# Selection flags of two row tiles side by side: three block turns a pair and a second indicator table

## What is computed

```
ub = sum(max(q * k_min, q * k_max))        # per query and chunk, chunks past the query masked
top_chunks = argsort(ub)[..., -6:]
scores = q @ k.T / 8                       # kept where the key's chunk is in top_chunks and key <= query
attn = softmax(scores);  x = attn @ v
```

## Time and profile before

| | |
|---|---|
| median of three runs | 276.93 us |
| the profiled execution | 276.81 us, its span 274.6 us |
| PE | 264.2 us busy, 96% of the span, 3630 matmuls |
| POOL | 223.4 us, 81% |
| DVE | 208.0 us, 76% |
| ACT | 151.2 us, 55% |

### The profile page before, as it was taken

The page is one execution under the profiler, slowest core; times in us unless marked ns, Lnnn a source line. Parts: engine busy times, 40 slices in busy tenths (PEclk is TensorE's granted clock), DMA queues, the critical chain, the costliest instruction groups (busy, mean ns, idle before and its releaser), DMA issues.

```text
span 274.6 us, 8756 instructions
## 1 busy us (share of the span) xinstructions
PE 264.2 (96%) x3630; PEld 167.8 (61%) x3630; DVE 208.0 (76%) x565; ACT 151.2 (55%) x228; POOL 223.4 (81%) x297
## 2 busy tenths in 40 slices
PE   7899999999999999999999999999999999987994
PEld 7556666565666565666665656757565657664663
DVE  5895787486969989758879897899799978962342
ACT  2295656565666565646584546465756576851220
POOL 6077999999999999998999999989899971726832
PEclk9999999999999999999999999999999999999999
DMA  9999999998999999999799979999998979511861
GB/s 149 181 151 145 272 207 168 328 195 168 180 183 178 171 175 182 171 174 184 128 188 169 202 129 196 155 200 175 181 345 189 299 167 201 106 40 50 156 137 62
DMA packets 154838, 48.31 MB, mean 176 GB/s; under 512 B 142447, under 2 KB 144358, under 8 KB 154768
## 3 DMA queue, kind: packets, MB, share of 16 engines
q1 hardware_dynamic: 141728, 28.73, 52.2%
q0 software_dynamic: 9936, 18.64, 38.6%
q10 hardware_dynamic: 3136, 0.39, 0.9%
HBM read 55.46 MB, written 11.01 MB: 242 GB/s over the span
## 4 chain that ended last, share of the span: by engine, by line
PE 89%; DVE 3%; ACT 2%; DMA 1%; issue 1%; another core or an unknown queue 1%; ACTq 1%; POOL 0%; DVEq 0%
PE OB L611 27%; PE SC L534 26%; PE SC L553 6%; PE OB L1357 4%; PE SC L1331 4%; PE MM L647 4%; PE OB L693 3%; PE MM L624 2%; PE MM L500 2%; PE SC L474 2%; PE MM L474 2%; DMA qn<-in_q_dram 1%; ACT EXB L562 1%; PE MM L686 1%; PE SC L794 1%
## 5 line engine op out<-in xcount | busy, mean ns | idle before, releaser
L562 ACT ACTIVATE EXB<-SC 128x1024 f32<-128x1024 f32 (+1 forms) x87 | 83.1, 966 | 38.4 <-PE SC L534 25.3
L586 POOL TENSOR_TENSOR ES<-ES,EXB 128x256 f32<-128x256 f32 (+1 forms) x98 | 96.9, 999 | 4.7
L534 PE MATMUL SC<-qT,kT 64*128 64x512 f32 (+3 forms) x476 | 86.3, 465 | 0.4 <-ACT EXB L562 0.3
L611 PE MATMUL OB<-EXB,vn 128*64 128x256 f32 (+3 forms) x704 | 72.6, 361 | 0.0
L611 PEld LDWEIGHTS OB<-EXB,vn 128*64 128x64 f32 x704 | 46.8, 137 | 23.1 <-issue 9.7
L534 PEld LDWEIGHTS SC<-qT,kT 64*128 64x128 f32 x476 | 39.3, 187 | 20.2 <-issue 14.5
L586 POOL TENSOR_TENSOR ES<-EXB 128x512 f32<-128x512 f32 (+1 forms) x29 | 45.2, 1560 | 2.4
L572 POOL TENSOR_SCALAR_AFFINE_SELECT EXB<-EXB 128x256 f32<-128x256 f32 x79 | 34.7, 450 | 3.8 <-ACT EXB L562 3.8
L619 ACT ACTIVATE oT<-OB 128x512 f32<-128x512 f32 (+1 forms) x32 | 15.7, 490 | 40.2 <-PE OB L611 40.2
L553 PE MATMUL SC<-unsT,ind 64*128 64x256 bf16 (+5 forms) x238 | 35.6, 295 | 0.0
L553 PEld LDWEIGHTS SC<-unsT,ind 64*128 64x128 bf16 x238 | 11.7, 94 | 18.5 <-issue 9.5
(11 more groups left out here) (266 smaller groups left out, 400.8 us busy)
## 6 DMA issues: line engine op xcount, KB each, us to landing
w1s<-in_moe_w_dram POOLq DMA_DIRECT2D x8, 1024.0 KB, 10.1
w2s<-in_moe_w_dram POOLq DMA_DIRECT2D x7, 1024.0 KB, 9.5
vn<-in_v_dram SPq DMA_DIRECT2D x32, 192.0 KB, 3.2
kn<-in_k_dram SPq DMA_DIRECT2D x62, 96.0 KB, 2.8
qn<-in_q_dram SPq DMA_DIRECT2D x62, 96.0 KB, 7.3
out_dram<-w1s SPq DMA_DIRECT2D x2, 1536.0 KB, 10.7
x_rows<-xp SPq DMA_DIRECT2D x16, 192.0 KB, 3.3
out_dram<-out_dram SPq DMA_DIRECT2D x1, 1536.0 KB, 12.2
```

The source lines that it names most:

```text
L534: op("pe", lambda: pe.matmul(o, kT[j][pr, ts(kt)], qT[j][pr, q0:q1], start=not flags and (not cols or cols[0] == 0), stop=bool(flags)), r= ...
L562: op("act", lambda: ac.activation(Ex(st, None, 0, W), src, ACTF.Exp, scale=SCALE), r=pk, w=[f"E{st}"])
L586: op(e, lambda: sy.queue[e].tensor_tensor(o, in0, in1, ALU.add), r=[f"E{s2}", f"E{first[0]}"] if first else [f"E{s2}"] + kt, w=kt)
L611: op("pe", lambda: pe.matmul(OB[pr, q0:q1], vn[s][:, kt, h, :], ex, start=(n == 0), stop=last), r=[f"vn{s}{h}", "ES0" if st is None else f ...
```

## The change

The flags of two row tiles stand side by side in one block. Within each head's 64 columns of a block, columns 0 to 23 hold a tile of queries 128 to 511, and columns 32 to 55 a tile of queries 512 to 767. So three blocks are turned instead of five, ACT copies 384 columns instead of 640 (for pair 0 in one copy instead of two), and DVE makes the flags in two comparisons, of three and of two tiles.

In the turned flags, queries from 512 on lie 32 partitions lower. Their product therefore needs a table whose rows are moved by 32: `ind2`, zero but for rows 32 to 63 of each half, which two transfers on SP copy from `ind`, one for each half. A piece of the triangle that crosses query 512 gets two products for each head instead of one. Three of the eight pieces do.

```diff
-                uns = al(pers, "uns", [128, NT - 1, 2, D], BF16)
-                unsT = [al(pers, "unsT", [128, (NT - 1) * 128], BF16) for _ in range(2)]
+                uns = al(pers, "uns", [128, NT // 2, 2, D], BF16)
+                unsT = [al(pers, "unsT", [128, NT // 2 * 128], BF16) for _ in range(2)]
...
+                ind2 = al(pers, "ind2", [128, NT * 128], BF16)
...
-                    return bass.AP((uns, unsT[0])[fb - 6], 0, [[(NT - 1) * 2 * D, 128], [1, Dm]])
+                    return bass.AP((ind, ind2)[fb - 6], 0, [[NT * 128, 128], [1, Dm]])
...
+                op("dve", lambda: ve.memset(ind2[:], 0.0), w=["ind2"])
...
-                    op("dve", lambda: ve.tensor_tensor(un, uv, thr, ALU.is_lt),
-                       r=["ubm", "M0"] + [f"top{t}{h}" for t in range(NT - 1) for h in range(2)], w=["uns"])
+                    for t0, n, half in ((0, NT // 2, 0), (NT // 2, NT // 2 - 1, 1)):
...
+                        un = bass.AP(uns, half * 32, [[NT // 2 * 2 * D, 128], [D, 2], [2 * D, n], [1, NCH]])
...
+                        op("dve", lambda: ve.tensor_tensor(un, uv, thr, ALU.is_lt),
...
-                    for t in range(NT - 1):
+                    for t in range(NT // 2):
...
-                    for c0, c1, key in ((0, 384, f"unsT{j}"), (384, (NT - 1) * 128, "unsTb")) if i == 0 else ((0, (NT - 1) * 128, f"unsT{j}"),):
-                        op("act", lambda: ac.activation(unsT[j][:, c0:c1], MB[:, c0:c1], ACTF.Copy), r=["MB"], w=[key])
+                    op("act", lambda: ac.activation(unsT[j][:], MB[:, 0:NT // 2 * 128], ACTF.Copy), r=["MB"], w=[f"unsT{j}"])
...
-                                op("pe", lambda: pe.matmul(o, ind[pr, ts(kt)], unsT[j][pr, b0 - 128:q1 - 128],
-                                                           start=early, stop=not early),
-                                   r=[f"ind{h}", f"unsT{j}"] + (["unsTb"] if i == 0 and st else []), w=pk, inc=last and not early)
+                            segs = [(lo, hi, t, n) for lo, hi, t, n in ((b0, min(q1, S // 2 + 128), ind, 0), (max(b0, S // 2 + 128), q1, ind2, 1)) if lo < hi]
+                            for g, (s0, s1, it, half) in enumerate(segs):
+                                for h in range(2):
...
+                                    m = 128 + half * (S // 2)
+                                    op("pe", lambda: pe.matmul(o, it[pr, ts(kt)], unsT[j][pr, s0 - m:s1 - m],
+                                                               start=early and g == 0, stop=not early and g == len(segs) - 1),
+                                       r=[f"ind{h}", f"indB{h}", f"unsT{j}"] if half else [f"ind{h}", f"unsT{j}"], w=pk,
...
                 load(2, "qk")
                 unselT(0)
                 score_mm(0, 2, None, (256, 512))
+                for h in range(2):
+                    op("sp", lambda: sp.dma_start(ind2[h * 64 + 32:h * 64 + 64, :], ind[h * 64:h * 64 + 32, :]), r=[f"ind{h}", "ind2"], w=[f"indB{h}"],
+                       dsem=f"d_ind{h}")
                 take_q(1)
                 take_k(1)
                 load(3, "qk")
```

More of the change, by code:

```diff
@@ L490, in bounds_out @@
                                r=["ubm"], w=[f"top{t}{h}"], inc=(t == NT - 2 and h == 1))
-                    thr = bass.AP(top8, 5, [[(NT - 1) * 16, 128], [8, 2], [16, NT - 1], [0, NCH]])
-                    un = bass.AP(uns, 0, [[(NT - 1) * 2 * D, 128], [D, 2], [2 * D, NT - 1], [1, NCH]])
-                    uv = bass.AP(MM, 192, [[1024, 128], [160, 2], [32, NT - 1], [1, NCH]])
-                    op("dve", lambda: ve.tensor_tensor(un, uv, thr, ALU.is_lt),
-                       r=["ubm", "M0"] + [f"top{t}{h}" for t in range(NT - 1) for h in range(2)], w=["uns"])
+                    for t0, n, half in ((0, NT // 2, 0), (NT // 2, NT // 2 - 1, 1)):
+                        thr = bass.AP(top8, 5 + t0 * 16, [[(NT - 1) * 16, 128], [8, 2], [16, n], [0, NCH]])
+                        un = bass.AP(uns, half * 32, [[NT // 2 * 2 * D, 128], [D, 2], [2 * D, n], [1, NCH]])
+                        uv = bass.AP(MM, 192 + t0 * 32, [[1024, 128], [160, 2], [32, n], [1, NCH]])
+                        op("dve", lambda: ve.tensor_tensor(un, uv, thr, ALU.is_lt),
+                           r=["ubm", "M0"] + [f"top{t}{h}" for t in range(NT - 1) for h in range(2)], w=[f"uns{half}"] + (["uns"] if half == 0 else []))
                 def unselT(i):
                     j = i % 2
-                    for t in range(NT - 1):
+                    for t in range(NT // 2):
                         op("pe", lambda: pe.transpose(MB[:, ts(t)], uns[:, t, :, :].rearrange("p a b -> p (a b)"), ident_bf[:]),
-                           r=["uns", "ident_bf"], w=["MB"], inc=(t == NT - 2))
-                    for c0, c1, key in ((0, 384, f"unsT{j}"), (384, (NT - 1) * 128, "unsTb")) if i == 0 else ((0, (NT - 1) * 128, f"unsT{j}"),):
-                        op("act", lambda: ac.activation(unsT[j][:, c0:c1], MB[:, c0:c1], ACTF.Copy), r=["MB"], w=[key])
+                           r=["uns", "uns0", "uns1", "ident_bf"], w=["MB"], inc=(t == NT // 2 - 1))
+                    op("act", lambda: ac.activation(unsT[j][:], MB[:, 0:NT // 2 * 128], ACTF.Copy), r=["MB"], w=[f"unsT{j}"])
                 def mid(i):
@@ L549, in scores @@
                             assert not early or b0 == q0
-                            for h in range(2):
-                                pr = slice(h * 64, h * 64 + 64)
-                                o = ps[:, pb + h * 512 + c + b0 - q0:pb + h * 512 + c + q1 - q0]
-                                op("pe", lambda: pe.matmul(o, ind[pr, ts(kt)], unsT[j][pr, b0 - 128:q1 - 128],
-                                                           start=early, stop=not early),
-                                   r=[f"ind{h}", f"unsT{j}"] + (["unsTb"] if i == 0 and st else []), w=pk, inc=last and not early)
+                            segs = [(lo, hi, t, n) for lo, hi, t, n in ((b0, min(q1, S // 2 + 128), ind, 0), (max(b0, S // 2 + 128), q1, ind2, 1)) if lo < hi]
+                            for g, (s0, s1, it, half) in enumerate(segs):
+                                for h in range(2):
+                                    pr = slice(h * 64, h * 64 + 64)
+                                    o = ps[:, pb + h * 512 + c + s0 - q0:pb + h * 512 + c + s1 - q0]
+                                    m = 128 + half * (S // 2)
+                                    op("pe", lambda: pe.matmul(o, it[pr, ts(kt)], unsT[j][pr, s0 - m:s1 - m],
+                                                               start=early and g == 0, stop=not early and g == len(segs) - 1),
+                                       r=[f"ind{h}", f"indB{h}", f"unsT{j}"] if half else [f"ind{h}", f"unsT{j}"], w=pk,
+                                       inc=last and not early and g == len(segs) - 1)
                             if early:
```

## The result

The changed kernel takes 290.86 us (median of 6 executions, 287.58 to 292.89) where the kernel before takes 276.88 on the same chip: a ratio of 1.043, with an interval of 1.035 to 1.050. The prediction was 285.0 with a range of 282.4 to 287.0. Direction and first cause were right, the size was not: 3 us are missing in the profiled execution, which took 287.89 us (span 285.6), and 3 more between that one and the median. The runs come from several chips, so each kernel is compared with the kernel before on its own chip.

A forecast was written before the change was run, and what follows sets the result against it. PE, busy 96% of the span and gapless from pair 1 on, was taken as the bound. Turns -1.7, split couples +0.2, wait +7.6 and clock +2.1 give +8.2 us on 276.81: 285.0, range 282.4 to 287.0.

The forecast's parts named there:

- The wait: PE in pair 0 waits for both table copies, queued on SP behind pair 2's loads: 8.1 us, net 7.6.
- The clock: After the wait in pair 0 PE's clock is at half speed for some microseconds: 2.1 us lost (1.4 to 2.9).
- Rival 2: Pair 0's wait alone costs time; the clock stays up or comes back at once: 282.9 us, chance 0.14.
- The split couples: Three more couples of products a pair on PE, same columns streamed: 0.2 us in all, upper end 4.5.
- Rival 3: Each split couple on PE costs a gap, 4.5 instead of 0.2 us in all: 289.3 us, chance 0.05.
- The turns: Two fewer turns a pair on PE save 0.115 us a pair, 1.7 us over 15 pairs; pair 0 gives nothing.
- rival 4: POOL or DVE becomes the bound, so PE's saving is not had: 286.5 us, chance 0.09.
- from pair 1 on, PE should again be gapless: Expected sign in the changed trace: after pair 0 PE runs without gaps, each pair about 0.1 us shorter.

The follow-up runs named there:

- The kernels with the copies elsewhere: Changed kernel with wide useless products at the start and the copies behind pair 3's loads (285.91 us, 1.045), ahead of the v loads (279.64 us, 1.019) or behind them (277.09 to 285.73).
- the kernel kept at work: Changed kernel with 36 more useless products of 512 columns ahead of the couple that waits for the copies: 284.15 us, 1.024 of the kernel before.
- the one with early copies: Changed kernel with the two table copies issued ahead of the v loads instead of behind pair 2's loads: 281.66 to 291.05 us in four executions.
- the shifted kernel before: Kernel before with 20 of its 62 useless start products replaced by 84 of 32 columns, 128 more PE instructions: 282.96 to 290.13 us in four executions.
- the kernel with early copies and wide useless products: Changed kernel with the copies ahead of the v loads and 16 useless start products of 512 columns for 62 of 128: 279.64 us, 1.019.

## Why the prediction was off

- **The wait: right.** Copies issued at 18.83 and 19.49 us (forecast 18.43 and 19.0), read at 21.02 and 21.43, 2.2 and 1.9 us later (forecast 2.4, and 21.4 for the second). The wait, 8.1 us by the forecast, is 7.7 us to the first copy and 8.1 to the second. First values 9.44 us late against 7.6 + 2.1 = 9.7. The kernels with the copies elsewhere bear out the place in the queue as the cause.
- **The clock: right.** 2.1 us forecast, 1.8 by the kernel kept at work. The step used the trace's own fall at the end and its rise at the start (5.8 us for 53 products is 0.109 us each, not 0.107, which changes nothing). Rival 2, the wait alone, falls: the granted clock was 0.50 from the wait to 25.87 us. The Trainium skill's rule ("TensorE: Matmul & The Clock Gate", Part 1) that idleness halves the rate held.
- **The split couples: right.** 0.29 us for 448 columns in one couple and in two. Rival 3 falls.
- **The turns: half had.** 0.1 us a pair forecast, so 1.4 over the 14 steps from pair 1 to pair 15, and 0.85 measured. The turns themselves give 0.10 a pair, but five of the 14 steps keep 0.03 or less. In the stretch of full work PE's weight loads for the row sums now wait longer for POOL (changed kernel, then the kernel before):

```profile
PEld MM L653 <- POOL ES L592: 1.8, 7, 0.3
```

```profile
PEld MM L647 <- POOL ES L586: 0.6, 3, 0.2
```

  That is rival 4 in part: 1.2 us of waits, most of them hidden behind products, where the prediction had argued from POOL's own 6 us of waiting that POOL had room for all of it. That these waits are the whole of the missing 0.55 us was not tested.
- **The step that failed: "from pair 1 on, PE should again be gapless".** The sum treated PE's program as always at hand. It comes in transfers of about 255 instructions, and the 128 sums, 256 instructions in 2.5 us, use one up faster than the next one came here. (Shown are the stop's going and coming with a shift of the program, and the transfer 2.2 to 2.5 us ahead of PE's going on; how far ahead of PE the transfers run is not.) The change adds products and removes turns, so the boundary falls elsewhere: 2.3 us of stop in the profiled execution, up to 3.5 in others, with a fall of the clock behind three of the four. Moved by 64 instructions, the changed kernel takes 285.27 us. Without its stop the profiled execution would be 285.6, so the sum of 285.0 was near for a kernel that doesn't stop (the turns' missing 0.55 accounts for most of the rest); neither the sum, nor a rival, nor the range had a place for the stop.

## What to carry over

Before pricing a copy, read which queue it stands in and what is issued ahead of it: two copies of 48 KB that were ready at 7 us landed at 21 because they were written behind eight loads, and an idle engine could have made them by 10.4. When a change alters the number of instructions on the busiest engine, look for its densest stretch and ask whether the supply of instructions keeps up there; shifting the program by a few dozen useless instructions is a cheap test, and for any kernel within a few per cent of another one it belongs in the comparison. Give the range a share for such stops, even where the engine is full in the trace of before.

## What the chip showed unexpectedly

- PE stopped 2.2 to 3.3 us for its own instructions in four profiles (the changed kernel twice, the one with early copies, the shifted kernel before), always after 120 of the 128 last sums, and in none of the kernels whose PE program was moved by 64, 72 or -92 instructions. DMA engines were full there (share 1.08 in the stretch from 238 to 242 us of the changed kernel), which may be why the transfer is late; that was not tested, and full queues alone don't do it: the data transfers' share was 110.6% during the same sums of the kernel before, which did not stop.
- The clock needs no long pause to fall. It stayed up through a stop of 2.16 us in the changed kernel and fell behind one of 2.16 in the kernel with the early copies; it fell for a wait of 1.55 us in pair 0, and only 3.1 us after the last product at the end of the kernel before. Behind one and the same wait of 1.6 to 1.7 us for DVE in the tail it fell in five profiles and stayed up in three, the kernel before among them. How long PE stood does not decide alone in these rows.
- A wait costs more than its length: 4.4 us for a late v delayed the later pairs by 7.4 us in the kernel with early copies and wide useless products, since PE then worked 5.3 us at half the clock.
